# Linear attention with its key-value sums turned round: v stationary on half-array tiles, key sums on GpSimd, leftover tokens in one tile

## Chip, cores and metric

One NeuronCore of a Trainium2 chip runs the whole kernel. The metric is the device time of one execution in microseconds (us); lower is better. The engines are named as in the profile: PE (TensorE), PEld (its weight loads), DVE (VectorE), ACT (ScalarE), POOL (GpSimd) and SP (SyncE, which issues the DMAs here).

## What is computed

Three layers follow each other over 8 batches of 576 tokens. The change is in the first, an attention with a feature map and no softmax (8 heads, head dimension 64, 128 features, so 256 exponentials for each token):

```python
def phi(x):
    proj = np.einsum('bhsd,df->bhsf', x, w_phi)
    proj = proj - np.max(np.abs(proj), axis=-1, keepdims=True)
    return np.concatenate([np.exp(proj), np.exp(-proj)], axis=-1)
q_p, k_p = (phi(q), phi(k))
kv = np.einsum('bhsf,bhsd->bhfd', k_p, v)
z = np.sum(k_p, axis=2)
num = np.einsum('bhsf,bhfd->bhsd', q_p, kv)
den = np.einsum('bhsf,bhf->bhs', q_p, z)[..., None] + 1e-06
attn = num / den
```

Its output, 512 wide, goes through two more layers. `_moe_ref` mixes each token with the one before it, then computes `sigmoid(xr @ w_r) * (relu(xk @ w_k)**2 @ w_v)`, with d_ff 1024. `_moe2_ref` is `h * sigmoid(conv3(h)) @ w_out` with `h = relu(x @ w_in)`.

## The kernel before, in words

`phase_1` computes the attention and the `_moe_ref` layer and `phase_2` the last layer. The change touches `phase_1` alone.

**Pairs and batches.** Attention works on two heads at a time, a pair p of 0 to 3; head h of the pair has its 64 channels on partitions 64h to 64h+63 of `qk`. `batches` runs the program in laps: first the attention of batch 0 alone (`first_attention_steps`), then seven laps that hold the attention of batch n+1 and the MoE layer of batch n (`iteration(True, True)`), and at last the MoE layer of batch 7. In a lap the MoE layer is cut into PE tiles of 12 matmuls each, named K, R, V- and V (K- and K+ are parts of a K tile), which are put between the attention's steps.

**The order is written out by a planner.** `iteration` walks through the steps of `attention_steps`. After each one it adds that step's entry of `PE_NS` to a clock and puts in MoE tiles worth `FILL_NS` of that step. Every engine walks through the same list and does its own part of each entry, in order. No engine overtakes: what stands later on an engine's list waits for what stands before it.

**The steps of one pair**, with the lines of the profile:
- E (`features_and_keys`, PE) multiplies q and k with `phi`. q comes out with features on partitions and tokens as columns, in `ps` (or `psm`); k with tokens on partitions, in five tiles of 128 tokens for each head, the fifth with 64 tokens and 64 zeros. `shift_keys` (DVE, L750 to L758) takes each key token's largest |value| and subtracts it, into `k_shift`.
- QT (`part_maxima`, DVE, L763 to L770) makes `q_part`, the maxima of q over 32 features at a time.
- EK (`exp_k`, ACT, L643 and L645): two exponentials, `k_exp` and, in place, `k_shift`.
- M (`turn_maxima`, PE, L515) transposes `q_part`. `spread_maxima` (DVE, L774 to L782) makes `max_blocks` of it.
- KV (`sum_kv`, PE): 20 matmuls with 128 exponentials stationary and 65 columns of `v_nat` moving, 64 of v and one of ones, whose column is z. `copy_kvz` (ACT, L657) brings the result to `kvz`.
- PICK (`subtract_maxima`, PE) waits for `max_blocks` and subtracts the maxima from q's features. `exp_q` (ACT, L652) makes four exponentials `q_exp`.
- DEN and NUM (PE) give denominator and numerator. ACT copies both out (L662, L667). RC (`spread_den`, `invert`, `repeat_den`) sends the denominator through DRAM and back, and DV (`divide`, DVE, L797) writes the attention's output `x` for this pair.
- XK, HK, LK and XR, HR, LR are the mixing of `x` and its split into high and low parts, on DVE (L809, L817), ACT (L688) and DVE (L825). K, R and V tiles have parts on ACT (L672 to L677, L693) and DVE (L830, L837) too.

Most matmuls of the profile have L459, the helper `mm`; they are told apart by their tiles. A float32 matmul leaves two records, so the 20 matmuls of KV are 40 records; a transpose or a float32r matmul leaves one.

Of the kernel before, what the change touches and what calls it, by code (L numbers as in the profile page):

```python
# [11 lines left out]
P = 128  # L12
# [12 lines left out]
VW = D + 1  # L25
# [159 lines left out]
def phase_1(nc, ctx, q, k, v, w_phi, mu_k, mu_r, w_k, w_v, w_r, y_scr, den_scr, w_in):  # L185
# [56 lines left out]
    zeroed, ident_ready, pick_made, pick_ready = sem("zeroed"), sem("ident_ready"), sem("pick_made"), sem("pick_ready")  # L242
    part_zeroed, own_made, tail_zeroed, banks_zeroed, x_zeroed = sem("part_zeroed"), sem("own_made"), sem("tail_zeroed"), sem("banks_zeroed"), sem("x_zeroed")
# [11 lines left out]
    kv_summed, kvz_copied = sem("kv_summed"), sem("kvz_copied")  # L255
# [29 lines left out]
    Q0, K_TAIL, Q_MAX, Q1 = 0, BANK + D, BANK + D + 2 * F, 2 * BANK - D  # L285
    CHUNKS = (((0, BANK), (BANK, S)), ((0, D), (D, S)))
# [60 lines left out]
    def _(sp):  # L347

        def load_qk(p, a):
# [3 lines left out]
            sp.dma_start(qk[:, p % 2, 0, 0:S], q[off, p] if reg is None else q[reg + off, p]).then_inc(q_loaded[p % 2], 16)  # L353
            await_(sp, k_projected, PAIRS, a, p - 1)
            sp.dma_start(qk[:, p % 2, 1, 0:S], k[off, p] if reg is None else k[reg + off, p]).then_inc(k_loaded[p % 2], 16)

        def load_v(p, a):
# [82 lines left out]
    def _(pool):  # L440
        nc.gpsimd.memset(v_nat[:], 0.0).then_inc(zeroed, 1)
# [10 lines left out]
        pool.wait_ge(zeroed, 1)  # L452
        nc.gpsimd.memset(v_nat[:, 0:4, :, D:D + 1], 1.0).then_inc(zeroed, 1)
        nc.gpsimd.memset(v_nat[0:TAIL, 4, :, D:D + 1], 1.0).then_inc(zeroed, 1)

    @block.tensor
    def _(pe):
# [10 lines left out]
        def features_and_keys(p, a):  # L468
# [701 lines left out]
```

## Time and profile before

| | us |
|---|---|
| median of 3 runs | 1399.35 (1394.55 to 1399.78) |
| the profiled execution's own time | 1397.19 |
| its span, first to last instruction | 1395.3 |
| busy: PE, DVE, ACT, POOL | 1333.8, 756.6, 599.2, 13.1 |

The span is the length of one profiled execution. Busy is the time in which an engine had an instruction under way. PE's matmuls are pipelined: a record's length is its latency, and what a stream of them costs is the distance from start to start.

### The profile page before, as it was taken

Reading aid. Unit: us, or ns where it says so; the run is one execution under the profiler, and the core shown is the slowest. Engines: PE = TensorE matmul, PEld = TensorE weight load, DVE = VectorE, ACT = ScalarE, POOL = GpSimd, SP = SyncE. Lnnn points to the kernel's source line nnn. Section 1 sums busy time; section 2 is a strip of 40 time slices with the busy share of each in tenths; the row PEclk is TensorE's granted clock in tenths of the full one; section 3 lists DMA queues with packets and bytes.
Section 4 is the critical chain, followed back from the end, with each engine's and each line's share of the span. In section 5 each row is a group of like instructions: output and inputs, shape, how many; then the busy total and the mean of one; then the engine's idle time right before and its main releaser. Section 6 shows DMA issues by size and latency. Waiting matters only on the chain. (4 is left out here: it accounts for less than half of the span.)

```text
span 1395.3 us, 25154 instructions
## 1 busy us (share of the span) xinstructions
PE 1333.8 (96%) x9720; PEld 1192.8 (85%) x9720; DVE 756.6 (54%) x1275; ACT 599.2 (43%) x1079; POOL 13.1 (1%) x18
## 2 busy tenths in 40 slices
PE   8779999999999999999999999998899999999998
PEld 7559898889888888888888888998798998998997
DVE  6557355545654544644565455451855755754853
ACT  3345445354353533534435344352533443533532
POOL 0000000000000000000000000000300000000000
PEclk9879999999999999999999999999999999999999
DMA  4421202202212111220221221221110110110101
GB/s 136 141 62 41 59 27 79 64 18 80 62 36 71 50 50 42 66 71 15 76 62 37 71 54 50 73 70 48 65 65 31 43 65 31 41 64 32 40 30 38
DMA packets 92657, 78.56 MB, mean 56 GB/s; under 512 B 62736, under 2 KB 71056, under 8 KB 91536
## 3 DMA queue, kind: packets, MB, share of 16 engines
q1 hardware_dynamic: 92560, 77.09, 18.4%
q8 instruction: 82, 1.34, 0.4%
q14 instruction: 15, 0.12, 0.0%
HBM read 57.75 MB, written 19.02 MB: 55 GB/s over the span
## 5 line engine op out<-in xcount | busy, mean ns | idle before, releaser
L459 PE MATMUL psm<-xk_hi,wk_hi 128*128 128x288 f32 x512 | 154.4, 302 | 14.5 <-issue 7.1
L982 PE MATMUL psh<-y_hi,win_hi 128*128 128x288 f32 x512 | 154.8, 302 | 13.4 <-ACT h L1067 9.0
L830 DVE TENSOR_TENSOR k_lo<-square,k_hi 128x288 fp32r<-128x288 f32 x128 | 58.5, 457 | 195.1 <-ACT square L677 194.8
L983 PE MATMUL psh<-y_lo,win_hi 128*128 128x288 f32 x512 | 153.1, 299 | 0.0
L459 PE MATMUL psm<-k_hi,wv_hi 128*128 128x288 f32 x512 | 152.8, 299 | 0.0
L984 PE MATMUL psh<-y_hi,win_lo 128*128 128x288 f32 x512 | 152.5, 298 | 0.0
L459 PE MATMUL psm<-xk_lo,wk_hi 128*128 128x288 f32 x512 | 152.2, 297 | 0.0
L459 PE MATMUL psm<-k_lo,wv_hi 128*128 128x288 f32 x512 | 152.0, 297 | 0.0
L459 PE MATMUL psm<-xk_hi,wk_lo 128*128 128x288 f32 x512 | 151.9, 297 | 0.0
L459 PE MATMUL psm<-k_hi,wv_lo 128*128 128x288 f32 x512 | 151.7, 296 | 0.0
L1125 DVE SCALAR_TENSOR_TENSOR conv<-h,taps,conv 128x576 f32<-128x576 f32 x64 | 55.2, 862 | 143.2 <-ACT conv L1069 143.2
L459 PEld LDWEIGHTS psm<-xk_hi,wk_hi 128*128 128x128 f32 x512 | 97.5, 190 | 18.2 <-issue 12.8
L982 PEld LDWEIGHTS psh<-y_hi,win_hi 128*128 128x128 f32 x512 | 98.0, 191 | 16.2 <-ACT h L1067 11.4
L984 PE MATMUL pso<-wout_hi,g_lo 128*128 128x512 f32 x256 | 101.1, 395 | 0.0
L982 PE MATMUL pso<-wout_hi,g_hi 128*128 128x512 f32 x256 | 101.0, 395 | 0.0
L983 PE MATMUL pso<-wout_lo,g_hi 128*128 128x512 f32 x256 | 101.0, 394 | 0.0
L672 ACT ACTIVATE relu<-psm 128x288 f32<-128x288 f32 x128 | 52.1, 407 | 108.6 <-PE psm L459 108.6
L459 PEld LDWEIGHTS psm<-k_hi,wv_hi 128*128 128x128 f32 x512 | 97.3, 190 | 1.3
L983 PEld LDWEIGHTS psh<-y_lo,win_hi 128*128 128x128 f32 x512 | 98.1, 192 | 0.3
L984 PEld LDWEIGHTS psh<-y_hi,win_lo 128*128 128x128 f32 x512 | 98.3, 192 | 0.0
L1067 ACT ACTIVATE h<-psh 128x576 f32<-128x576 f32 x64 | 41.8, 653 | 131.3 <-DVE gated L1113 92.8
L459 PEld LDWEIGHTS psm<-xk_lo,wk_hi 128*128 128x128 f32 x512 | 97.4, 190 | 0.6
(130 smaller groups left out, 2900.4 us busy)
## 6 DMA issues: line engine op xcount, KB each, us to landing
v_nat<-in_v SPq DMA_DIRECT2D x32, 320.0 KB, 3.6
qk<-in_q SPq DMA_DIRECT2D x32, 288.0 KB, 3.3
qk<-in_k SPq DMA_DIRECT2D x32, 288.0 KB, 3.7
den<-den_scr SPq DMA_DIRECT2D x64, 144.0 KB, 3.0
y_scr<-y SPq DMA_DIRECT2D x64, 144.0 KB, 2.0
y<-y_scr SPq DMA_DIRECT2D x8, 1152.0 KB, 5.6
out<-rows SPq DMA_DIRECT2D x32, 256.0 KB, 2.0
stage<-in_moe_w_in SPq DMA_DIRECT2D x4, 512.0 KB, 3.2
```

The costliest lines, as they stand in the source:

```text
L459: return nc.tensor.matmul(o, lhsT, rhs, start=first, stop=last, skip_group_check=True)
L672: nc.scalar.activation(relu[:, i % 2, :], psm[:, UNIT["K", n, i] % 3, 0:HALF], ACT.Relu).then_inc(k_relu, 1)
L830: nc.vector.tensor_tensor(k2_lo[:, i, :], square[:, i % 2, :], k2_hi[:, i, :].bitcast(F32), ALU.subtract).then_inc(k2_lo_ready, 1)
L982: nc.tensor.matmul(o, wh, xh, start=first, stop=False, skip_group_check=True)
L983: nc.tensor.matmul(o, wh, xl, start=False, stop=False, skip_group_check=True)
L984: return nc.tensor.matmul(o, wl, xh, start=False, stop=last, skip_group_check=True)
L1067: nc.scalar.activation(two(h[:, j % 2, 1:1 + S]), psh[:, j % 2, :, 0:HALF], ACT.Relu, scale=0.5).then_inc(h_ready, 1)
L1125: nc.vector.scalar_tensor_tensor(out=conv[:, j % 2, :], in0=h[:, j % 2, 0:S], scalar=taps[:, 0, j:j + 1], in1=conv[:, j % 2, :], op0=ALU.m ...
```

## The change

KV is turned round. `v_nat` now is stationary, 64 columns of one head, and both sets of exponentials (2 x 128 columns) move; head 0 writes partitions 0 to 63 and head 1 partitions 64 to 127 of one PSUM bank. The result has v's channels on partitions, so ACT copies it to `kvt` (new `copy_kvt`), three PE transposes turn it back (new step T, `turn_kv`), and ACT copies those to `kvz`. z no longer is a 65th column: POOL adds the eight full key tiles down to two (new `sum_keys`, four adds a pair) and eight matmuls with a column of ones finish it. The 64 leftover tokens of both heads share one tile (9 tiles in place of 10), which shortens both exponentials from 1280 to 1152 columns. q's columns are cut 288/288 and 224/352 in place of 512/64 and 64/512. `exp_q` is done in two halves, head 0 at PICK, head 1 behind the new `kvz` copy at T. The planner's costs and fills are new.

```diff
-PE_NS = {"E": 2800, "M": 150, "PICK": 700, "KV": 4500, "DEN": 1200, "NUM": 2200,
+PE_NS = {"E": 2800, "M": 150, "PICK": 600, "T": 350, "KV": 3000, "DEN": 1200, "NUM": 2200,
-FILL_NS = {"E": 1600, "QT": 1600, "EK": 3200, "PICK": 3200, "NUM": 1600}
+FILL_NS = {"E": 1600, "QT": 1600, "EK": 4800, "T": 3200, "NUM": 1600}
...
-    CHUNKS = (((0, BANK), (BANK, S)), ((0, D), (D, S)))
+    CHUNKS = (((0, HALF), (HALF, S)), ((0, 2 * BANK - Q1), (2 * BANK - Q1, S)))
...
+        def sum_keys(p, a):
+            for e in range(2):
+                tiles = k_exp[:, e, 0:KEYS - 1, :].rearrange("s (g y) f -> s g y f", y=2)
+                await_(pool, k_exp_ready, 2 * PAIRS, a, 2 * p + e + 1)
+                await_(pool, z_summed, 2 * PAIRS, a, 2 * p + e)
+                nc.gpsimd.tensor_tensor(z_pairs[:], tiles[:, :, 0, :], tiles[:, :, 1, :], ALU.add).then_inc(z_paired, 1)
+                halves = z_pairs[:].rearrange("s (h x) f -> s h x f", x=2)
+                await_(pool, z_paired, 2 * PAIRS, a, 2 * p + e + 1)
+                await_(pool, kv_summed, PAIRS, a, p)
+                nc.gpsimd.tensor_tensor(z_sums[:, e, :, :], halves[:, :, 0, :], halves[:, :, 1, :], ALU.add).then_inc(z_summed, 1)
...
         def features_and_keys(p, a):
-            key_tile(0, TT - 1).then_inc(shared_bank, 1)
-            feature_chunk(1, 1, True)
-            feature_chunk(0, 0, True)
-            await_(pe, shared_bank, 3 * PAIRS, a, 3 * p + 1)
-            key_tile(1, TT - 1).then_inc(shared_bank, 1)
             key_tile(0, 0)
             key_tile(1, 0)
-            await_(pe, shared_bank, 3 * PAIRS, a, 3 * p + 2)
+            key_tail(0)
+            key_tail(1).then_inc(shared_bank, 1)
+            await_(pe, shared_bank, 2 * PAIRS, a, 2 * p + 1)
+            feature_chunk(0, 0, True)
+            feature_chunk(1, 1, True)
...
         def sum_kv(p, a):
             await_(pe, v_loaded, 16 * PAIRS, a, 16 * (p + 1))
-            for e, src in enumerate((k_exp, k_shift)):
-                await_(pe, k_exp_ready, 2 * PAIRS, a, 2 * p + e + 1)
+            await_(pe, k_exp_ready, 2 * PAIRS, a, 2 * p + 2)
+            own = [slice(D * h, D * h + D) for h in range(2)]
+            for t in range(TT - 1):
                 for h in range(2):
-                    for t in range(TT):
-                        last = mm(ps1[:, 0, VW * (2 * h + e):VW * (2 * h + e) + VW], src[:, h, t, :], v_nat[:, t, h, :],
-                                  t == 0, t == TT - 1)
+                    tile = (TT - 1) * h + t
+                    mm(kv_turned()[own[h], :, :], v_nat[:, tile, :], k_exp[:, :, tile, :], t == 0, False)
+            for h in range(2):
+                mm(kv_turned()[own[h], :, :], v_nat[own[h], KEYS - 1, :], k_exp[own[h], :, KEYS - 1, :], False, True)
+            await_(pe, z_summed, 2 * PAIRS, a, 2 * p + 2)
+            for h in range(2):
+                for e in range(2):
+                    mm(z_row(h, e), ones[:], z_sums[:, e, h, :], True, False)
+            for h in range(2):
+                for e in range(2):
+                    last = mm(z_row(h, e), ones[own[h], :], k_exp[own[h], e, KEYS - 1, :], False, True)
             last.then_inc(kv_summed, 1)
+
+        def turn_kv(p, a):
+            await_(pe, kvt_copied, PAIRS, a, p + 1)
+            for i in range(3):
+                last = nc.tensor.matmul(ps1[:, 1, P * i:P * i + P], kvt[:, P * i:P * i + P], ident[:], start=True, stop=True,
+                                        is_transpose=True, skip_group_check=True)
+            last.then_inc(kvz_turned, 1)
...
         def copy_kvz(p, a):
-            await_(act, kv_summed, PAIRS, a, p + 1)
+            await_(act, kvz_turned, PAIRS, a, p + 1)
             await_(act, attended, PAIRS, a, p)
```

**What moves on DVE.** In pair 1 of a steady lap this is DVE's list from the reciprocal of the denominator to the first step of `spread_maxima` before:

```order
L791 RECIPROCAL den_cols<-den_cols 128x9
L763 STREAM_TRANSPOSE q_turn<-ps 128x576 x2
L766 TENSOR_REDUCE q_part<-q_turn 128x2x18
L770 COPY q_part<-q_part 128x64
L817 SCALAR_TENSOR_TENSOR mix<-diff,mu,x 128x288 x4
L837 SCALAR_TENSOR_TENSOR y<-gate,psm 128x288
L797 TENSOR_TENSOR x<-num,den 128x576
L825 TENSOR_TENSOR xr_lo<-mix,xr_hi 128x864
L774 TENSOR_REDUCE q_max<-ps 128x32
```

The same stretch of DVE's list now:

```order
L843 RECIPROCAL den_cols<-den_cols 128x9
L869 SCALAR_TENSOR_TENSOR mix<-diff,mu,x 128x288 x3
L815 STREAM_TRANSPOSE q_turn<-ps 128x576 x2
L818 TENSOR_REDUCE q_part<-q_turn 128x2x18
L822 COPY q_part<-q_part 128x64
L869 SCALAR_TENSOR_TENSOR mix<-diff,mu,x 128x288
L889 SCALAR_TENSOR_TENSOR y<-gate,psm 128x288
L877 TENSOR_TENSOR xr_lo<-mix,xr_hi 128x864
L849 TENSOR_TENSOR x<-num,den 128x576
L877 TENSOR_TENSOR xr_lo<-mix,xr_hi 128x288
L889 SCALAR_TENSOR_TENSOR y<-gate,psm 128x288
L826 TENSOR_REDUCE q_max<-ps 128x32
```

Three mixes stand ahead of the transposes of q, and a second `xr_lo` and a second `y` ahead of `q_max`.

**What moves on ACT.** The exponentials of pair 1 and what stands around them before:

```order
L693 ACTIVATE gate<-psm 128x288 x3
L643 ACTIVATE k_exp<-k_shift 128x1280
L645 ACTIVATE k_shift<-k_shift 128x1280
L688 ACTIVATE xr_hi<-mix 128x864
L688 ACTIVATE xr_hi<-mix 128x288
L657 ACTIVATE kvz<-ps 128x260
L652 ACTIVATE q_exp<-ps 128x576 x4
L662 ACTIVATE den_rows<-ps 128x576
```

And now:

```order
L743 ACTIVATE gate<-psm 128x288 x2
L738 ACTIVATE xr_hi<-mix 128x864
L689 ACTIVATE k_exp<-k_exp 128x1152
L691 ACTIVATE k_exp<-k_exp 128x1152
L738 ACTIVATE xr_hi<-mix 128x288
L702 ACTIVATE kvt<-ps 128x384
L697 ACTIVATE q_exp<-ps 128x576 x2
L707 ACTIVATE kvz<-ps 128x384
L697 ACTIVATE q_exp<-ps 128x576 x2
L712 ACTIVATE den_rows<-ps 128x576
```

`xr_hi` of 864 columns, which waits for the three mixes, stands ahead of the exponentials, and the copy to `kvz` stands behind half of `q_exp`.

**What moves on PE** where no MoE tile lies between, in the attention of batch 0, from M of pair 0 into E of pair 1, before:

```order
L515 MATMUL ps<-ident,q_part 128x128
L459 MATMUL ps<-v_nat,k_exp 128x65 x10
L459 MATMUL ps<-v_nat,k_shift 128x65 x10
L459 MATMUL ps<-max_blocks,pick 128x512
L459 MATMUL ps<-max_blocks,pick 128x64 x2
L459 MATMUL psm<-phi,qk 128x128
```

And now:

```order
L544 MATMUL ps<-ident,q_part 128x128
L486 MATMUL ps<-k_exp,v_nat 64x256 x10
L486 MATMUL ps<-z_sums,ones 1x128 x4
L486 MATMUL ps<-k_exp,ones 1x128 x4
L486 MATMUL ps<-max_blocks,pick 128x288 x2
L486 MATMUL ps<-max_blocks,pick 128x224
L486 MATMUL ps<-max_blocks,pick 128x352
L578 MATMUL ps<-ident,kvt 128x128 x3
L486 MATMUL ps<-phi,qk 128x128 x2
```

The transposes stand between PICK and the next E, and the next E waits for `kvz`, which is copied behind them.

## Rows read from the trace of the kernel before

**Rows 1.** The page, engines: busy us, share of the span, instructions.

```profile
PE 1333.8 (96%) x9720; PEld 1192.8 (85%) x9720; DVE 756.6 (54%) x1275; ACT 599.2 (43%) x1079; POOL 13.1 (1%) x18
```

**Rows 2.** Busy time by stretch: length, then each engine's busy us; PEclk; DMA.

```profile
329.70:444.40 114.70, 111.54 (x902) 99.31 (x901) 59.99 (x112) 51.37 (x101) 0.00 (x0) 1.00 0.20 58
444.40:561.00 116.60, 113.48 (x903) 100.92 (x901) 59.97 (x112) 51.76 (x101) 0.00 (x0) 0.99 0.19 51
```

**Rows 3.** Groups by form, PE: busy us, mean ns; idle before.

```profile
L459 PE MATMUL ps<-v_nat,k_exp 128*128 128x65 f32 x640 | 76.8, 275 | 0.0
```

**Rows 4.** Timeline of PE, pair 0 of a lap: start, length.

```profile
444.65 0.37 PE L459 MATMUL ps<-phi,qk 64*128 64x128 f32 x1
...
454.54 0.33 PE L515 MATMUL ps<-ident,q_part 128*128 128x128 f32 x1
454.72 2.44 PE L459 MATMUL ps<-v_nat,k_exp 128*128 128x65 f32 x20
...
459.20 0.93 PE L459 MATMUL ps<-max_blocks,pick 128*128 128x512 f32 x4
459.97 0.29 PE L459 MATMUL psm<-xk_hi,wk_hi 128*128 128x288 f32 x1
...
463.24 3.25 PE L459 MATMUL ps<-q_exp,kvz 128*1 128x64 f32 x32
```

**Rows 5.** Waits, whole span: us in total, times, longest.

```profile
PE ps L459 <- DVE max_blocks L782: 12.2, 15, 5.0
PEld ps L515 <- DVE q_part L770: 6.0, 21, 0.3
```

**Rows 6.** Timeline of PE (first row) and DVE, pair 1 of a lap.

```profile
353.47 0.37 PE L459 MATMUL ps<-phi,qk 64*128 64x128 f32 x1
...
362.17 0.20 DVE L770 COPY q_part<-q_part 128x64 f32<-128x64 f32 x1
362.28 1.80 DVE L817 SCALAR_TENSOR_TENSOR mix<-diff,mu,x 128x288 f32<-128x288 f32 x4
...
364.48 0.76 DVE L797 TENSOR_TENSOR x<-num,den 128x576 f32<-128x576 f32 x1
365.15 1.05 DVE L825 TENSOR_TENSOR xr_lo<-mix,xr_hi 128x864 fp32r<-128x864 f32 x1
...
366.88 0.76 DVE L782 TENSOR_TENSOR max_blocks<-own_block,q_max_split 128x576 fp32r<-128x576 f32 x1
```

**Rows 7.** Timeline of ACT, pair 1 (first row) and pair 0.

```profile
361.32 1.28 ACT L645 ACTIVATE k_shift<-k_shift 128x1280 f32<-128x1280 f32 x1
...
454.89 0.39 ACT L672 ACTIVATE relu<-psm 128x288 f32<-128x288 f32 x1
...
455.99 0.39 ACT L672 ACTIVATE relu<-psm 128x288 f32<-128x288 f32 x1
```

**Rows 8.** Timeline of PE and DVE, pair 3 of a lap.

```profile
516.46 0.37 PE L459 MATMUL ps<-phi,qk 64*128 64x128 f32 x1
...
530.44 0.76 DVE L782 TENSOR_TENSOR max_blocks<-own_block,q_max_split 128x576 fp32r<-128x576 f32 x1
```

**Rows 9.** Timeline of POOL and DVE in the last layer.

```profile
977.85 0.82 DVE L1128 SCALAR_TENSOR_TENSOR conv<-h,taps,conv 128x576 f32<-128x576 f32 x1
...
981.60 2.42 POOL L1093 TENSOR_TENSOR wout_lo<-stage,wout_hi 128x1024 fp32r<-128x1024 f32 x1 [0.65 <-ACT wout_hi L1038]
...
981.60 3.02 DVE L1128 SCALAR_TENSOR_TENSOR conv<-h,taps,conv 128x576 f32<-128x576 f32 x1
```

**Rows 10.** Busy time of two stretches around PICK of pair 1; columns as rows 2.

```profile
480.00:483.40 3.40, 2.70 (x23) 2.52 (x23) 3.02 (x7) 0.39 (x1) 0.00 (x0) 1.00 0.13 43
483.40:486.80 3.40, 3.40 (x15) 3.30 (x15) 0.00 (x0) 2.28 (x4) 0.00 (x0) 0.50 0.42 96
```

**Rows 11.** Timeline of ACT, batch 0, pair 0.

```profile
22.06 0.39 ACT L657 ACTIVATE kvz<-ps 128x260 f32<-128x260 f32 x1 [3.14 <-PE ps L459]
...
23.29 2.26 ACT L652 ACTIVATE q_exp<-ps 128x576 f32<-128x576 f32 x4
```

More of the change, by code:

```diff
@@ L49, in attention_steps @@
 def attention_steps():
-    return [(s, p) for p in range(PAIRS) for s in ("E", "QT", "EK", "M", "KV", "PICK", "DEN", "NUM")]
+    return [(s, p) for p in range(PAIRS) for s in ("E", "QT", "EK", "M", "KV", "PICK", "T", "DEN", "NUM")]
 def first_attention_steps():
@@ L62, in first_attention_steps @@
         steps += [("E", p), ("QT", p), ("EK", p)] + before("DEN", "NUM") + [("WARM", p)] + before("RC")
-        steps += [("M", p), ("KV", p), ("PICK", p)] + before("DV")
+        steps += [("M", p), ("KV", p), ("PICK", p), ("T", p)] + before("DV")
     p = PAIRS - 1
@@ L213, in phase_1 @@
     max_blocks = sb_att("max_blocks", [P, TOK, 32], F32R)
-    k_shift = sb_att("k_shift", [P, 2, TT, F])
-    k_exp = sb_att("k_exp", [P, 2, TT, F])
-    pick_f = k_exp[:, :, 0, :]
+    k_exp = sb_att("k_exp", [P, 2, KEYS, F])
+    z_pairs, z_sums = sb_att("z_pairs", [P, 4, F]), sb_att("z_sums", [P, 2, 2, F])
+    pick_f = k_exp[:, 0, 0:2, :]
     q_exp = sb_att("q_exp", [P, 2, 2, S])
-    kvz = sb_att("kvz", [P, 2, 2, VW])
+    kvt = sb_att("kvt", [P, 3 * F])
+    kvz = sb_att("kvz", [P, 3, P])
     num = sb_att("num", [P, S])
@@ L283, in second_of @@
         return reg is None and off == 1
-    Q0, K_TAIL, Q_MAX, Q1 = 0, BANK + D, BANK + D + 2 * F, 2 * BANK - D
-    CHUNKS = (((0, BANK), (BANK, S)), ((0, D), (D, S)))
+    K_TAIL, Q0 = 0, BANK - HALF
+    Q1 = Q0 + S
+    Q_MAX = Q1 + S
+    CHUNKS = (((0, HALF), (HALF, S)), ((0, 2 * BANK - Q1), (2 * BANK - Q1, S)))
     def att_psum(p, a):
@@ L450, in _, with work @@
                                     pattern=[[-1, TOK]], channel_multiplier=1).then_inc(own_made, 1)
-        pool.wait_ge(zeroed, 1)
-        nc.gpsimd.memset(v_nat[:, 0:4, :, D:D + 1], 1.0).then_inc(zeroed, 1)
-        nc.gpsimd.memset(v_nat[0:TAIL, 4, :, D:D + 1], 1.0).then_inc(zeroed, 1)
+        def sum_keys(p, a):
[8 more added lines that the diff above has]
+                nc.gpsimd.tensor_tensor(z_sums[:, e, :, :], halves[:, :, 0, :], halves[:, :, 1, :], ALU.add).then_inc(z_summed, 1)
+        def work(m, a, steps):
+            if a is not None:
+                for p in range(PAIRS):
+                    sum_keys(p, a)
+        batches(pool, work)
     @block.tensor
@@ L545, in sum_den @@
                         row = 32 * (2 * h + e)
-                        mm(q_cols(1, p, a)[row:row + 1, cols], kvz[:, h, e, D:D + 1], q_exp[:, e, h, cols], True, True)
+                        mm(q_cols(1, p, a)[row:row + 1, cols], kvz[:, 2, row:row + 1], q_exp[:, e, h, cols], True, True)
         def attend(p, a):
@@ L553, in attend @@
                     for h in range(2):
-                        last = mm(q_cols(0, p, a)[D * h:D * h + D, cols], kvz[:, h, e, 0:D], q_exp[:, e, h, cols], e == 0, e == 1)
+                        last = mm(q_cols(0, p, a)[D * h:D * h + D, cols], kvz[:, e, D * h:D * h + D], q_exp[:, e, h, cols], e == 0, e == 1)
             last.then_inc(attended, 1)
@@ L608, in work @@
                     sum_kv(step[1], a)
+                elif kind == "T":
+                    turn_kv(step[1], a)
                 elif kind == "DEN":
@@ L701, in work @@
                 elif kind == "PICK":
-                    exp_q(step[1], a)
+                    exp_q(0, step[1], a)
                 elif kind == "KV":
+                    copy_kvt(step[1], a)
+                elif kind == "T":
                     copy_kvz(step[1], a)
+                    exp_q(1, step[1], a)
                 elif kind == "NUM":
```

90 lines of the change are left out of this document (50 added, 40 removed).

## The prediction

> **What bounds the kernel now.** I read the page's busy shares first: PE is busy 96% of the span [rows 1], so a change is worth what it takes off PE's list, less what it adds to PE's waits. Then busy time by stretch. The seven laps that hold attention are alike; an undisturbed one takes 114.7 us, and two of the seven take 116.6 [rows 2]. Then PE's timeline in one lap. From M on, KV's 40 records take 4.48 us (454.72 to 459.20), PICK 0.77, two MoE tiles 3.27 (so 1.6 us a tile), DEN and NUM together 3.25 with the latency of the last record [rows 4]. A record of KV is 275 ns long [rows 3] but the next starts 0.11 us later: it has 65 columns moving and 128 stationary, and the pace is that of the weight load. Last, the waits: PICK waited for `max_blocks` 15 times in `ps`, 12.2 us in all, and M for `q_part` 21 times by 0.3 us [rows 5]. So the maxima of q already end as late as KV in half of the pairs. What the change does to that chain counts as much as what it does to KV.
>
> **KV on PE.** DEN and NUM have the new form (32 or 64 columns of the array, two or four matmuls side by side). They send 1728 columns one after another (576 for DEN, 1152 for NUM) in about 3.05 us net of the last latency, 1.77 ns a column [rows 4]. New KV sends 4 x 256, then 256 for the leftover tile, then 128 and 128 for z: 1536 columns, 2.7 us, and I add 0.2 for changes of form: 2.9 in place of 4.48. PICK loses its two narrow matmuls: 0.6 in place of 0.77. T adds three transposes, each a record like M's, which is 0.18 us ahead of KV [rows 4]: 0.40. DEN and NUM have more even chunks: -0.05. E has a new exposed wait on its own tails and shorter tails: 0, with 0.1 either way. So PE's own list gets 1.6 + 0.15 - 0.4 + 0.05 = 1.4 us shorter for each pair. The bounds for KV are 2.7 (no change of form costs anything) and 3.9 (below).
>
> The Trainium skill (TensorEngine Tiling, Tiling Modes, Key Properties) says that a change of tiling mode, not of tile alone, drains the engine. New KV changes its tile shape five times between M and PICK. By the rows such a step costs 0.1 or so; by the rule, priced with the 275 ns of a record, KV would be 3.9 us. That would show only in pair 3, where KV ends last, and make the time some 6 us longer.
>
> **The chain of the maxima.** It decides when PICK can start. I walk DVE's new list from the start of E. Before, PICK starts 14.55 us after E in pair 0 [rows 4], 14.2 in pair 1 (366.88 + 0.76 - 353.47, [rows 6]) and 14.7 in pair 3 [rows 8]; pair 2 is bound by KV as pair 0 is, with one tile less: 14.1. Now every pair has one more MoE tile between E and M, so M is 1.25 to 1.6 later.
> - Pair 0: the added tile is K7. Its ACT part queues behind the exponentials, and K tiles go through ACT at 1.10 us each (454.89 to 455.99, [rows 7]); its `k_lo` stands ahead of `q_max`. `max_blocks` ends at 15.4.
> - Pair 1: three mixes (0.43 us each, 4 in 1.80, [rows 6]) now stand ahead of the transposes of q, so `q_part` ends 1.5 later, at 10.4. Then one mix, `y`, `xr_lo` 1.0, `x` 0.7, `xr_lo` 0.4, `y` 0.4, and 1.5 from `q_max` to the end of `max_blocks`: 15.2. The exponentials now wait for `xr_hi`, which waits for the mixes; they end at 10.8 (before: 361.32 + 1.28 - 353.47 = 9.1, [rows 7]).
> - Pair 2: as pair 0, with `x` in the queue: 14.95. Pair 3: only R tiles are added, no `k_lo` is ahead, and `x` waits for its denominator until about 11.5: `max_blocks` ends at 13.8, and KV at 14.0 decides.
>
> **What GpSimd does to that chain.** This is the cost that I weigh most. In the last layer a POOL op of 1024 columns takes 2.42 us, and a DVE instruction that starts with it takes 3.02 us where it otherwise takes 0.82 [rows 9]: it is held for as long as POOL works, less 0.2. The held instruction reads two tensors of SBUF, as do `k_lo`, `mix`, `xr_lo`, `x` and `max_blocks`. The new adds take 2 x (1.25 + 0.65) = 3.8 us a pair by that row, from the end of the first exponential on. In pair 0 most of it falls where DVE waits for ACT anyway: 15.5 in place of 15.4. In pair 2 it costs 0.8: 15.75. In pair 1 DVE has no slack: the adds run from 9.6 on between its ops, each holding the next one: about +2.3, 17.5. In pair 3 they are over before `x`.
>
> [...]
>
> **Sum of a lap.** PICK later by 0.95 + 3.3 + 1.65 - 0.7 = +5.2. One tile more done ahead of it in each pair: 4 x 1.6 = -6.4. Behind PICK, T less the small gains: +0.2 a pair, +0.8. At the lap's end six V tiles in place of eight R and V tiles hide the last denominator, `x` and the split; I find `xk_lo` ready just when K+ wants it: +0.1 (up to +0.8). That is -0.3 to -0.5 a lap, -3 for seven. The 2.1 us of extra length in two laps is a stretch of 3.4 us at half the clock (1.2 GHz) after PE stood still for 0.7 us behind the weight-bound KV [rows 10]; new KV keeps the array busier, and I count these as gone: -4.
>
> **Batch 0** has no tiles between steps. E of the next pair waits for `kvz`, which so far was copied before PICK (22.06, ahead of `q_exp` at 23.29, [rows 11]). Now ACT does half of `q_exp` first, 1.1 us of the 2.26 for four, then the copy, 0.4, after 0.25 for the signal; less T's own place the next E starts 1.7 us later, three times, and the last DEN 0.4: +5.3. Bounds 2 and 8; none of it can be a gain, since PICK there waits for the denominators of the pair before, not for KV whose longest wait was 5.0 us [rows 5].
>
> Against the profiled execution's own 1397.2 (2.2 below the median, within the runs' spread): 1397.2 - 3 - 4 + 5.3 = 1395.5, so **1396**, own range 1386 to 1406. What the edit takes off PE is given back as waits for `max_blocks`.
>
> **Rivals.** A measurement of this kernel tells a change from none at about 0.5%, 7 us.
> - *The adds hold nobody up.* PICK at 15.4, 15.2, 14.95, 14.0: +2.1 - 6.4 + 0.9 = -3.4 a lap. 1397.2 - 24 - 4 + 5.3 = **1375**. For it: POOL's op could be short in so small a size. Against: the held instruction of [rows 9].
> - *It does what it says.* The waits stay as they are and 1.4 us go from each of 28 pairs: -39, with batch 0: **1360**. For it: PE is 96% busy. Against: one more K tile's work on ACT and DVE stands ahead of `max_blocks`.
> - *Slower: PE cools in front of PICK 1.* With KV done at 14.1 and PICK at 17.5, PE stands still 3.4 us in each lap. After 0.7 us of standing still the granted clock was 0.50 for the next 3.4 us, which costs 1.9 [rows 2, 10]. If that follows in all seven laps where it came in two before, it adds 5 x 1.9 to 1397.2 - 3 + 5.3: **1409**. The point is a wait of some 2 us or more behind dense work; against it, waits of 0.3 to 0.6 us before PICK left the clock whole in the other laps.
>
> **Chances.** Forecast 0.45, adds harmless 0.22, as it says 0.10, cooling 0.23. The forecast's own range lies 0.15 under 1392.4, 0.28 within 0.5%, 0.02 over 1406.4; cooling 0.14 over and 0.09 within. Faster 0.47, same 0.37, slower 0.16. The range reaches from 1366 (most of the harmless case) to 1412 (most of the cooling one).
>
> **What would show it.** KV: from M to z some 2.9 us on PE. Adds: z_pairs about 1.25 us, and beside them `xr_lo` or `k_lo` longer than 2 us. PICK's wait for `max_blocks`: 1.3, 3.4, 1.8 and 0 us in pairs 0 to 3. Batch 0: E of pairs 1 to 3 waits for ACT's `kvz`. A `max_blocks` that ends before KV in pairs 0 to 2, or DVE's ops at their old lengths beside POOL, would make the forecast wrong; so would a KV over 4 us.

## The result, and the profile after

The changed kernel takes **1442.47 us** (median of 4 runs, 1440.22 to 1446.7), the kernel before beside it 1396.95 (4 runs, 1392.69 to 1399.78): ratio 1.0332, 95% interval 1.029 to 1.0374. That is 3.3% slower, and 46 us from the prediction of 1396, outside its range. The profiled execution is one of 1440.22 us; the one of before took 1397.2.

The page's busy shares of the kernel after, to be laid beside [rows 1]:

```profile
PE 1328.0 (92%) x9688; PEld 1130.2 (79%) x9688; DVE 788.8 (55%) x1274; ACT 609.0 (42%) x1111; POOL 163.3 (11%) x144
```

TensorE (PE) was busy 6 us less and its span is 43 us longer, so it stood still 49 us more; part of what is left of its busy time ran at the lower clock (below). VectorE (DVE) is 32 us busier with one instruction less; no operation was added there, so its instructions became longer.

The first four laps after; columns as [rows 2]:

```profile
113.57:236.40 122.83, 115.52 (x899) 95.87 (x898) 63.48 (x113) 52.38 (x104) 18.73 (x16) 0.93 0.16 47
236.40:354.05 117.65, 109.71 (x897) 90.83 (x897) 64.87 (x113) 52.69 (x105) 17.94 (x16) 0.99 0.17 51
354.05:474.00 119.95, 111.24 (x897) 92.04 (x897) 63.85 (x112) 52.41 (x105) 17.94 (x16) 0.97 0.17 52
474.00:593.30 119.30, 111.37 (x898) 92.41 (x898) 64.46 (x113) 53.03 (x105) 18.45 (x16) 0.97 0.18 54
```

A lap is 3 to 8 us longer than 114.7, and its clock is rarely whole. The 43 us lie so: the first lap starts at 113.6 where it started at 101.2 (batch 0, +12.4); six laps take 717.9 where they took 691.3 (+26.7); the seventh with what follows until the last layer +5.8; the last layer -1.7.

PE's timeline in pair 0 of a lap (start, length, idle before and its releaser), with E at 354.05, beside [rows 4]:

```profile
354.05 0.86 PE L486 MATMUL ps<-phi,qk 64*128 64x128 f32 x8
...
357.29 0.40 PE L486 MATMUL psm<-xk_hi,wk_hi 128*128 128x288 f32 x1
...
365.73 0.27 PE L544 MATMUL ps<-ident,q_part 128*128 128x128 f32 x1
365.93 2.53 PE L486 MATMUL ps<-k_exp,v_nat 128*64 128x256 f32 x20
368.39 0.40 PE L486 MATMUL ps<-z_sums,ones 128*1 128x128 f32 x8
368.72 0.40 PE L486 MATMUL ps<-k_exp,ones 64*1 64x128 f32 x8
370.08 0.82 PE L486 MATMUL ps<-max_blocks,pick 128*128 128x288 f32 x4 [0.97 <-DVE max_blocks L834]
370.74 0.49 PE L578 MATMUL ps<-ident,kvt 128*128 128x128 f32 x3
370.98 0.38 PE L486 MATMUL psm<-xr_hi,wr_hi 128*128 128x288 f32 x1
```

KV with z runs from 365.93 to its last start at about 368.85, 2.9 us as forecast; PICK takes 0.66 until the transposes, these 0.24 until the next tile: the edit does on PE what it says. But the first tile comes 3.24 us after E's start, where it came 2.77 after it before (444.65 to 447.42), and PICK stands 0.97 us idle.

PE's waits over the whole span, beside [rows 5]:

```profile
PE ps L486 <- DVE max_blocks L834: 32.8, 22, 4.7
PE ps L486 <- POOL z_sums L474: 15.1, 11, 1.5
PE psm L486 <- DVE xk_lo L877: 10.8, 6, 3.3
```

DVE and POOL (GpSimd) in pair 1 of the same lap, where E starts at 379.28; before: [rows 6]:

```profile
389.75 0.72 DVE L822 COPY q_part<-q_part 128x64 f32<-128x64 f32 x1
390.39 0.51 DVE L869 SCALAR_TENSOR_TENSOR mix<-diff,mu,x 128x288 f32<-128x288 f32 x1
390.82 0.44 DVE L889 SCALAR_TENSOR_TENSOR y<-gate,psm 128x288 f32<-128x288 f32 x1
391.18 1.22 DVE L877 TENSOR_TENSOR xr_lo<-mix,xr_hi 128x864 fp32r<-128x864 f32 x1
392.33 1.82 DVE L849 TENSOR_TENSOR x<-num,den 128x576 f32<-128x576 f32 x1
394.07 0.97 DVE L877 TENSOR_TENSOR xr_lo<-mix,xr_hi 128x288 fp32r<-128x288 f32 x1
...
396.08 0.76 DVE L834 TENSOR_TENSOR max_blocks<-own_block,q_max_split 128x576 fp32r<-128x576 f32 x1
```

```profile
389.12 1.29 POOL L470 TENSOR_TENSOR z_pairs<-k_exp 128x512 f32<-128x512 f32 x1 [20.84 <-ACT k_exp L689]
390.57 0.92 POOL L474 TENSOR_TENSOR z_sums<-z_pairs 128x256 f32<-128x256 f32 x1 [0.16 <-POOL z_pairs L470]
391.63 1.90 POOL L470 TENSOR_TENSOR z_pairs<-k_exp 128x512 f32<-128x512 f32 x1
393.61 1.12 POOL L474 TENSOR_TENSOR z_sums<-z_pairs 128x256 f32<-128x256 f32 x1
```

Read the two by their ends. `q_part` ends at 390.47, just behind the first `z_pairs` (390.41); `x` at 394.15, 0.62 behind an add's end (393.53); the second `xr_lo` at 395.04, 0.31 behind the next one's (394.73). `x` takes 1.82 us where it took 0.76 [rows 6]. The adds are held as well: the second `z_pairs` starts while the long `xr_lo` still runs (to 392.40) and needs 1.90 where the first needs 1.29.

`x` isn't the costliest of them over the whole run. These are VectorE's groups after (count, busy us, mean ns), then the copy in a run without adds (run 1 below):

```profile
L822 DVE COPY q_part<-q_part 128x64 f32<-128x64 f32 x32 | 21.2, 661 | 1.1
L849 DVE TENSOR_TENSOR x<-num,den 128x576 f32<-128x576 f32 x32 | 35.9, 1123 | 33.1 <-DMA den<-den_scr 32.9 <-issue 0.2
```

```profile
L821 DVE COPY q_part<-q_part 128x64 f32<-128x64 f32 x32 | 6.3, 196 | 1.1
```

The small copy alone is 14.9 us longer, `x` 11.7, `k_lo` 5.7 and `xr_lo` 4.9.

What TensorE's clock does there: the same columns for stretches of 3.4 us.

```profile
392.70:396.10 3.40, 1.34 (x22) 0.36 (x20) 3.30 (x7) 0.49 (x1) 1.95 (x2) 0.99 0.02 6
396.10:399.50 3.40, 2.60 (x11) 2.56 (x12) 0.74 (x1) 1.22 (x3) 0.00 (x0) 0.50 0.45 130
399.50:402.90 3.40, 3.40 (x16) 3.40 (x15) 0.00 (x0) 1.45 (x3) 0.00 (x0) 0.50 0.02 5
402.90:406.30 3.40, 3.40 (x36) 1.98 (x36) 0.45 (x1) 0.00 (x0) 0.00 (x0) 1.00 0.13 43
```

PE is busy for 1.34 of 3.40 us while it waits for `z_sums` and then `max_blocks`; the clock is then at 1.2 GHz (0.50) for 6.8 us, with 11 and 16 instructions, and 36, of another mix, in the next stretch at the whole clock. From the start of the first lap to that of the seventh 44 us pass at 0.50, before the change 10.

### The profile page after: what moved, and what is told of

The parts are those of the page before. It is cut to its first block and busy times, and to the rows that moved or that the text cites. A ratio compares the mean times of both kernels' runs of the same rounds, so it can differ in the third digit from the quotient of the medians.

```text
span 1438.4 us, 25420 instructions
## 1 busy us (share of the span) xinstructions
PE 1328.0 (92%) x9688; PEld 1130.2 (79%) x9688; DVE 788.8 (55%) x1274; ACT 609.0 (42%) x1111; POOL 163.3 (11%) x144
## 5 line engine op out<-in xcount | busy, mean ns | idle before, releaser
L486 PE MATMUL psm<-xk_hi,wk_hi 128*128 128x288 f32 x512 | 159.7, 312 | 21.2 <-DVE xk_lo L877 10.8
L470 POOL TENSOR_TENSOR z_pairs<-k_exp 128x512 f32<-128x512 f32 x64 | 91.6, 1432 | 762.8 <-ACT k_exp L689 758.2
L486 PE MATMUL psm<-k_hi,wv_hi 128*128 128x288 f32 x512 | 157.2, 307 | 0.0
L486 PE MATMUL psm<-xk_lo,wk_hi 128*128 128x288 f32 x512 | 156.1, 305 | 0.0
L882 DVE TENSOR_TENSOR k_lo<-square,k_hi 128x288 fp32r<-128x288 f32 x128 | 64.3, 502 | 118.2 <-ACT square L727 118.2
L486 PEld LDWEIGHTS psm<-xk_hi,wk_hi 128*128 128x128 f32 x512 | 101.3, 198 | 28.6 <-issue 18.6
L889 DVE SCALAR_TENSOR_TENSOR y<-gate,psm 128x288 f32<-128x288 f32 x64 | 28.7, 449 | 137.8 <-PE psm L486 137.2
L486 PE MATMUL ps<-phi,qk 64*128 64x128 f32 (+1 forms) x632 | 91.0, 309 | 11.6 <-DVE pick L790 6.3
L486 PEld LDWEIGHTS psm<-xk_lo,wk_hi 128*128 128x128 f32 x512 | 101.4, 198 | 0.0
L486 PEld LDWEIGHTS psm<-xk_hi,wk_lo 128*128 128x128 f32 x512 | 101.1, 198 | 0.0
```

What stands on the lines that cost most here:

```text
L470: nc.gpsimd.tensor_tensor(z_pairs[:], tiles[:, :, 0, :], tiles[:, :, 1, :], ALU.add).then_inc(z_paired, 1)
L486: return nc.tensor.matmul(o, lhsT, rhs, start=first, stop=last, skip_group_check=True)
L882: nc.vector.tensor_tensor(k2_lo[:, i, :], square[:, i % 2, :], k2_hi[:, i, :].bitcast(F32), ALU.subtract).then_inc(k2_lo_ready, 1)
L889: nc.vector.scalar_tensor_tensor(out=y[:, i % 2, :], in0=gate[:, i, :], scalar=1.0, in1=psm[:, UNIT["V", n, i] % 3, 0:HALF], op0=ALU.add, ...
```

## The experiments

After the result I had this theory: the adds on GpSimd hold VectorE back, so PICK waits, and PE's clock falls behind the longer waits; E and batch 0 add their own. Each is tried apart. Runs 1 to 7 are one execution each, and so is the first time of run 9; the kernel before, executed with them, took 1396.5 us beside runs 1 to 4 and 1393.8 beside runs 5, 6, 7 and 9. Such a time is compared below with the fastest execution of the changed kernel, 1440.2, unless it says otherwise; executions of one kernel here differ by 5 to 8 us. An idle matmul is one whose result nobody reads.

**1. No adds at all** (`e1_no_adds`). `z_sums` is set to ones once, so the key sums lack all but the leftover tokens; nobody waits for GpSimd.

```diff
-                for p in range(PAIRS):
-                    sum_keys(p, a)
+                pass
...
-            await_(pe, z_summed, 2 * PAIRS, a, 2 * p + 2)
```

> The changed kernel with GpSimd's four adds a pair left out: z_sums is filled with ones once and nobody waits for it, so z is wrong; every matmul stays. Theory H (the adds hold VectorE's instructions, so max_blocks is late): in pair 1 of a steady lap max_blocks ends at 15.2 to 15.6 us after the start of E in place of 17.6, in pair 2 at 15.3 in place of 16.3, in pair 0 hardly earlier; k_lo and xr_lo return to their old lengths (0.46 and 1.05 us); a lap is 2.5 to 3 us shorter by that alone, and most of the eleven half-clock stretches of the laps go with the shorter waits: 1405 to 1415 us in all. Rival W (only TensorE's wait for z_summed costs): max_blocks ends where it did, pair 1 still has PICK at 17.6, and the time stays over 1430.

Measured: 1403.05 us. DVE in pair 1 (E at 366.44):

```profile
376.91 0.20 DVE L821 COPY q_part<-q_part 128x64 f32<-128x64 f32 x1
...
377.82 1.05 DVE L876 TENSOR_TENSOR xr_lo<-mix,xr_hi 128x864 fp32r<-128x864 f32 x1
378.79 0.75 DVE L848 TENSOR_TENSOR x<-num,den 128x576 f32<-128x576 f32 x1
379.45 0.45 DVE L876 TENSOR_TENSOR xr_lo<-mix,xr_hi 128x288 fp32r<-128x288 f32 x1
...
380.94 0.76 DVE L833 TENSOR_TENSOR max_blocks<-own_block,q_max_split 128x576 fp32r<-128x576 f32 x1
```

The same instructions are back at 0.20, 1.05, 0.75 and 0.45. `max_blocks` ends 15.83, 15.25, 15.43 and 14.21 us after E in pairs 0 to 3, with the adds 15.98, 17.56, 16.25 and 14.73. Without the adds the kernel is 37 us shorter (1405 to 1415 us was expected); a lap takes 114.3, and from the first lap to the start of the seventh 14 us pass at 0.50 in place of 44.

**2. Adds made, nobody waits for them** (`e7_adds_unread`). The adds run as in the changed kernel; PE multiplies a constant tile, so the key sums again lack most tokens. PE's wait for `z_sums` goes, VectorE's hold stays. So that nothing is overwritten, ScalarE and VectorE wait for the adds in PE's place, at the next exponentials and at `x` (not shown).

```diff
-            await_(pe, z_summed, 2 * PAIRS, a, 2 * p + 2)
...
-                    mm(z_row(h, e), ones[:], z_sums[:, e, h, :], True, False)
+                    mm(z_row(h, e), ones[:], z_fixed[:, e, h, :], True, False)
```

> The changed kernel with the adds made as before, but TensorE reads a constant in place of their result and doesn't wait for them, so z is wrong. Theory H: VectorE is held as before, max_blocks ends at 17.6 us in pair 1, the time is within 5 us of the changed kernel's 1440 us. Rival W (TensorE's wait for the sums is what costs): the time falls to that of the run without adds.

Measured: 1441.49 us, as slow as the changed kernel's 1440 to 1447. `max_blocks` ends 15.98, 17.56, 16.25 and 14.74 us after E, to 0.01 us as with the wait. The wait for `z_sums` (15.1 us in the table of waits) costs nothing that can be told: PICK behind it waits longer for the maxima, 54.2 us in all where it was 38.3. It is the hold.

**3. The changed kernel kept busy** (`e4_warm`). 23 idle matmuls of the identity in each lap, put where PE waits in pairs 0 to 2.

```diff
+            for _ in range({0: 4, 1: 6, 2: 7}.get(p, 0) if not first_of(a) else 0):
+                mm(ps1[:, 1, 0:P], ident[:], ident[:], True, True)
             await_(pe, blocks_ready, PAIRS, a, p + 1)
```

(and 6 more in pair 1 ahead of the wait for `z_sums`.)

> The changed kernel with 23 idle matmuls of 128 columns a steady lap put where TensorE stands still (6 ahead of the wait for the sums and 6 ahead of PICK in pair 1, 7 ahead of PICK in pair 2, 4 in pair 0); they write a bank that nobody reads. Theory C (part of the loss is the half clock that follows the long waits): most of the eleven half-clock stretches in the laps (each 3.4 us long, some 1.7 us lost) go, and the kernel is 10 to 18 us faster: 1422 to 1430. Rival (the clock doesn't matter, the waits are the whole loss): no faster than 1437, or slower by the matmuls themselves, where a wait was shorter than they are.

Measured: 1427.12 us, 13 less, with the maxima where they were. The third and fourth lap, columns as [rows 2]:

```profile
354.44:471.58 117.14, 114.04 (x944) 94.82 (x943) 64.14 (x112) 52.73 (x106) 18.53 (x16) 1.00 0.17 47
471.58:589.34 117.76, 115.23 (x943) 96.30 (x943) 64.50 (x112) 52.47 (x104) 17.94 (x16) 0.99 0.19 53
```

PE does some 46 records more than in the same laps above and is done 2.8 and 1.5 us sooner, while the clock reads 1.00 and 0.99 where it read 0.97. So some 13 of the 43 us are clock, and that is a lower bound: from the first lap to the start of the seventh 20 us still pass at 0.50, where it was 44, and 10 before the change.

**4. Tails earlier inside E** (`e3_e_order`).

```diff
             key_tile(0, 0)
-            key_tile(1, 0)
             key_tail(0)
             key_tail(1).then_inc(shared_bank, 1)
+            key_tile(1, 0)
+            key_tile(0, 1)
+            key_tile(1, 1)
             await_(pe, shared_bank, 2 * PAIRS, a, 2 * p + 1)
             feature_chunk(0, 0, True)
             feature_chunk(1, 1, True)
-            key_tile(0, 1)
-            key_tile(1, 1)
```

> The changed kernel with another order inside E: the two 64x64 tails second to fourth and three more key tiles behind them, so that the wait for their bank is covered by key tiles before q's first chunks. Theory E (the exposed wait and the changes of tile form make E 3.14 us from first to last start, 0.47 more than before): E falls to 2.8 to 2.9 us, and 32 of them give 8 to 12 us: 1428 to 1433. Rival (E is hidden behind VectorE's chain to PICK, so its length is free): E is shorter and the time stays within 3 us of 1440.

Measured: 1438.99 us, 1.2 below the fastest run of the changed kernel, above the 1428 to 1433 that I expected and within the rival's 3 us. From its first to its last instruction (by their starts) E takes 2.89 us in place of 3.03, half of what I expected; before the change it took 2.57. The rival's reason doesn't hold all the same: `max_blocks` and PICK come 0.14 us earlier behind the start of E in pairs 0 to 2, and an undisturbed pair is 0.13 to 0.14 us shorter (pair 0: 25.10 for 25.24). Over 32 pairs that is 4 us; in this execution 51 us of the six laps ran at 0.50 where it was 44, which takes about as much. So the place of the tails is less than a third of E's 0.46; the rest lies in the form of its other instructions (chunks of 288, 288, 352 and 224 columns among the tiles in place of 512 and 64, narrow tails), which I didn't separate.

**5. The key sums on TensorE** (`f1_z_on_pe`), correct arithmetic with no adds: 16 narrow matmuls a pair in place of 4.

```diff
-            await_(pe, z_summed, 2 * PAIRS, a, 2 * p + 2)
-            for h in range(2):
-                for e in range(2):
-                    mm(z_row(h, e), ones[:], z_sums[:, e, h, :], True, False)
+            for t in range(TT - 1):
+                for h in range(2):
+                    for e in range(2):
+                        mm(z_row(h, e), ones[:], k_exp[:, e, (TT - 1) * h + t, :], t == 0, False)
```

> The changed kernel with GpSimd's adds given back to TensorE: z sums all eight full key tiles with 16 matmuls of 128 columns, four side by side, in place of 4 of the added-up tiles; GpSimd does nothing in the laps. By the run without adds (1403.05 us, laps of 114.2), and 0.65 us more of matmuls a pair, which only pair 3 and part of pair 0 show since PICK comes later than KV in the others: 1403 to 1412 us. If the adds' price were something else than VectorE being held (memory traffic of GpSimd, the wait), this would tell nothing new; if it is above 1425, the extra matmuls are on the path in all pairs and the account of the waits is wrong.

Measured: 1406.75 us. All key sums by PE cost 3.7 us more than leaving them out (one execution each, within the spread of executions), the adds on GpSimd 36 us more than this (median against this time). Four narrow matmuls lie side by side in different columns of the array: their records start 0.007 us apart. PE is busy 22 us more than in run 1 (1336.5 for 1314.1): in pair 3, where no maxima are waited for, PICK comes 0.66 us later (15.25 for 14.59), in pairs 0 to 2 where it came before. The extra work fills PE's wait for the maxima and is nearly free for that reason.

**6. Batch 0's copy first** (`f2_kvz_first`): version 5, and in batch 0 `kvz` is copied ahead of the exponentials of q.

```diff
-                elif kind == "PICK":
+                elif kind == "PICK" and not first_of(a):
                     exp_q(0, step[1], a)
...
                     copy_kvz(step[1], a)
+                    if first_of(a):
+                        exp_q(0, step[1], a)
```

> The kernel with z on TensorE, and in batch 0 alone the copy to kvz ahead of both halves of q_exp on ScalarE. Theory B (in batch 0 the next E waits for kvz, which stands behind half of q_exp): E of pairs 1, 2 and 3 starts 1.1 us earlier after PICK each, and with the half clock it sits in up to twice that: the first lap starts 3 to 6 us earlier than in the run with z on TensorE, the laps stay. Rival: E is held by something else (the loads, num_copied) and nothing moves.

Measured: 1399.80 us, 7 below version 5; the first lap starts at 109.6 in place of 113.6, and the other 3 us are within the spread of executions. ACT's rows of the changed kernel, batch 0, pair 0, beside [rows 11], show what was undone:

```profile
23.07 0.49 ACT L702 ACTIVATE kvt<-ps 128x384 f32<-128x384 f32 x1 [4.07 <-PE ps L486]
23.45 1.05 ACT L683 ACTIVATE wk_hi<-mix 128x1024 fp32r<-128x1024 f32 x1
24.40 1.18 ACT L697 ACTIVATE q_exp<-ps 128x576 f32<-128x576 f32 x2
25.46 0.50 ACT L707 ACTIVATE kvz<-ps 128x384 f32<-128x384 f32 x1
```

A piece of weights (`wk_hi`, 1.05 us) also stands ahead of the copy of `kvz`. I hadn't counted it. This run leaves it where it is. E of the next pair starts at 26.0, before at 22.7.

**7. One tile later** (`f3_late_tile`): version 5 with `"EK": 3200, "T": 4800`, one MoE tile from ahead of M to behind the transposes.

> The kernel with z on TensorE and the planner's fill before M at 3200 ns as in the kernel before, with the tile put behind T (4800). My account: in each pair M comes 1.57 us earlier, but max_blocks only 0.4 to 1.2 us earlier (its K tile's work on ScalarE and VectorE is 1.1, one y is 0.4), so a pair gets 0.4 to 1.1 us longer where max_blocks decides: laps 1 to 3 us longer, 1410 to 1420. Rival F (the table that puts one more tile ahead of M is part of the loss): laps 1 to 3 us shorter, under 1403.

Measured: 1428.09 us, 21 slower than version 5 and 8 above what I expected. In pairs 0 and 3 PICK comes 1.0 to 1.2 us earlier, in pairs 1 and 2 0.4, for a tile of 1.6 that now lies behind it: PE waits for the maxima instead. In pairs 1 and 2 M isn't what delays them most; that it is VectorE's own queue is my reading of the rest.

**8. One tile earlier** (`h2_early_tile`): version 9 below with `"EK": 6400, "T": 1600`, and the copy of `kvz` first in every batch.

> The last version (key sums on TensorE, no adds, tails earlier in E, idle matmuls in batch 0), with one MoE tile moved from behind the transposes to ahead of M, and ScalarE's copy for kvz first in every batch. Theory (TensorE waits 0.2 to 1.0 us for the maxima ahead of PICK, and VectorE's own queue, not M, sets when they are ready): a tile of 1.6 us ahead of M moves PICK by about 0.9, and kvz is ready 1.5 us after the transposes, so DEN follows the one tile left there with 0.1 to 0.3 of waiting: 0.4 us less for each of 28 pairs, 1392 - 11 = 1381 us. Rival (the maxima move with M as they did when the tile was moved the other way, by 1.1 us in pair 0): PICK is 1.1 to 1.6 later and the wait for kvz is added, 1392 to 1400 us.

Measured: 1436.18 us (4 runs; ratio 1.0282, 1.0263 to 1.0301). I expected 1381, the rival 1392 to 1400: both missed. PE and, below, ACT in pair 1 (E at 375.3):

```profile
391.98 0.81 PE L485 MATMUL ps<-max_blocks,pick 128*128 128x288 f32 x4
392.67 0.55 PE L579 MATMUL ps<-ident,kvt 128*128 128x128 f32 x3
395.96 2.27 PE L485 MATMUL ps<-q_exp,kvz 128*1 128x224 f32 x24 [1.16 <-ACT q_exp L700]
```

```profile
393.25 0.49 ACT L710 ACTIVATE kvz<-ps 128x384 f32<-128x384 f32 x1 [0.64 <-PE ps L579]
393.64 2.27 ACT L700 ACTIVATE q_exp<-ps 128x576 f32<-128x576 f32 x4
```

PICK no longer waits here, but DEN does: I had costed its wait by `kvz` and forgotten the four exponentials of q (2.27 us), which DEN needs too. Over the span PE waits for them 28 times, 33.9 us in all, which is most of the 43 us that this costs over version 9. PICK is 1.3 to 1.6 us later behind E in pairs 1 to 3, as the rival had it, and 2.5 later in pair 0 (18.23 for 15.73). With two tiles behind the transposes DEN doesn't wait for `q_exp` in the laps, with one it does.

**9. All of it** (`f4_all`): version 6 with E's order of run 4, and idle matmuls in PE's waits of batch 0 (18 ahead of PICK of pairs 1 and 2, 6 behind the transposes). `i1_all_again` is the same kernel, timed; `i2_no_warm` has no idle matmuls.

> z on TensorE, the copy to kvz first in batch 0, the other order inside E, and in batch 0 idle matmuls where TensorE stands still (18 before PICK of pairs 1 and 2, 6 behind T). By the parts: 1403 to 1410 less 3 to 6 (kvz) less 4 (E) less 3 to 6 (full clock in batch 0): 1388 to 1400, as fast as the kernel before or slightly faster. If it stays above 1405, batch 0's length is not a matter of clock and copies.

> The version that ran once at 1392.2 us, timed: the changed kernel with the key sums on TensorE (no adds), ScalarE's copy for kvz ahead of the exponentials of q in batch 0, the tails earlier in E, and idle matmuls in batch 0. One theory: its single time stands for it, 1392 within 2, and a ratio to the kernel before of 0.997. Rival: that run was a good one (the granted clock was whole in six of the seven laps), and its median lies at 1394 to 1398, no faster than before.

> The same without the idle matmuls of batch 0. In the version with the copy first alone (1399.8) batch 0 had 37 us of half clock and E took 5.4 us there, and the first attention lap began at 109.6; with the tails earlier and the idle matmuls at 103.4. Theory (the idle matmuls did it): without them the lap begins at 108.5 to 109.5, and the time is 1397 to 1399. Rival (in batch 0 VectorE's queue is the bound, as the kernel before with idle matmuls suggests, whose lap began no earlier for them: 103.4 against 101.2): the lap begins at 104 to 106 and the time is 1393 to 1395.

Measured: 1392.17 in one execution; timed again, **1393.6** (12 runs, 1391.24 to 1396.67) against 1395.46 for the kernel before (23 runs), ratio 0.9987, interval 0.9972 to 1.0001. Without the idle matmuls 1396.81 (10 runs), ratio 1.0009, interval 0.9993 to 1.0024. The first lap starts at 103.4 and 104.5 with them, at 109.7 without. So in this kernel they give 3 us (their means are 3.0 apart, with an interval of 1.2 to 4.8), and the whole edit, freed of what it cost, is worth nothing that can be told. In the profiled executions six laps take 686.6 us where they took 691.3 before the change, and the first starts 3.3 later.

The page of `i1_all_again`:

```profile
PE 1334.2 (96%) x10564; PEld 1141.2 (82%) x10564; DVE 749.6 (54%) x1274; ACT 609.2 (44%) x1111; POOL 12.5 (1%) x16
```

VectorE is at 749.6 us, 39 below the changed kernel (run 1, without the adds, has 749.7): that much of its busy time was the hold.

**10. The control** (`h1_before_warm`): the kernel before, with idle matmuls in batch 0 alone.

```diff
+            for _ in range(16 if first_of(a) and p in (1, 2) else 0):
+                mm(ps1[:, 1, 0:P], ident[:], ident[:], True, True)
             await_(pe, blocks_ready, PAIRS, a, p + 1)
```

(and 3 behind PICK of pairs 0 to 2.)

> The kernel before, with nothing of the change, and idle matmuls (128x128) in TensorE's waits of batch 0 alone: 16 ahead of PICK of pairs 1 and 2, 3 behind PICK of pairs 0 to 2. It asks whether the last version's gain (1392.2 us with the key sums on TensorE, ScalarE's copy first, the tails earlier in E and idle matmuls in batch 0) owes anything to the change. Theory (it owes nothing, what was gained there is the clock of batch 0, which the kernel before can have as well): half-clock stretches of batch 0 go from 31 us in all to some 15, E of batch 0 takes 2.6 us where it took 4.2, and 1396 - 7 = 1389 us. Rival (the change's form of KV keeps its own advantage, the clock of batch 0 matters little in the kernel before): 1396 within 2, above the 1392 of that version.

Measured: 1400.47 us (10 runs; ratio 1.0027, 1.0012 to 1.0043), 4 us slower than the kernel before, where I expected 1389 and the rival 1396. Its clock rose (0.97 over batch 0, before 0.86), E took 2.57 us there where it took 4.2, and the first lap still began 2.2 us later. PE's waits of its first 110 us:

```profile
PE psm L459 <- DVE xk_lo L829: 9.5, 2, 6.2
```

What the clock gave comes back as a wait for `xk_lo` (before 5.2 us in all). I read this as VectorE's work setting the length of batch 0, not PE's; no run moved that work, so it is argued and not shown.

## Why the prediction was wrong, step by step

Per lap PICK is later by 1.5, 3.4, 2.2 and 0 us in pairs 0 to 3, where "PICK later by 0.95 + 3.3 + 1.65 - 0.7" stood. The mechanism that the forecast weighed most, the hold by GpSimd, was right. What failed are four terms of its sum: the length of E (put at 0), the lap's end, the clock (counted as a gain) and batch 0.

- **KV, PICK, T on PE: right.** 2.9, 0.66 and 0.24 us by starts, where 2.9, 0.6 and 0.40 stood. The ten matmuls of 256 columns (20 records) with their change of form fit in 2.46 us; where the form changes inside KV the next start comes 0.31 us later in place of 0.22, so about 0.1 a change. The Trainium skill (TensorEngine Tiling, Key Properties) says that a change of tiling mode drains the engine. If it does here, the drain costs that 0.1 and not a record's 0.275 (priced so, five changes on 2.7 would be 4.1; the prediction's 3.9 is a slip).
- **The chain of the maxima: right within 0.4.** 15.4 / 15.2 / 14.95 without the hold; without adds, run 1 has 15.83 / 15.25 / 15.43, of which 0.46 is E. Less that, pairs 0 and 2 are met; pair 1 is 14.8, and the 15.2 that stood there fitted only because the missing E made up for it.
- **The hold by GpSimd: right in mechanism and size, and the rival "harmless" fell.** Forecast 0.1, 2.3 and 0.8 us; the difference to run 1 is 0.15, 2.3 and 0.8. The sign that I gave for it, an `xr_lo` or `k_lo` of over 2 us, didn't come: the longest are 1.22 and 0.82, and the longest `x` is 1.82. Only what is left of the add counts: no `k_lo` started with more than 0.51 us of an add to go, no `x` with more than 1.20. `y`, with one operand in PSUM, kept its 0.44 us and the reductions theirs, but the copy of `q_part`, with one input and that in SBUF, took 0.72 in place of 0.20, and over the run it is the largest part of the hold, 14.9 of 39 us; I had not counted it. The Trainium skill (SBUF — State Buffer, Who interferes with whom) says that a copy can enter a mode that takes the ports shared with GpSimd, and that a reduction on trn2 never contends. The trace agrees: the copies that started under an add took 0.68 us or more, the nine reductions their usual time.
- **E: the step that failed first.** "0, with 0.1 either way" is +0.46 us by its starts, in every pair at the whole clock. It shifts the chain of the maxima too, since all of it is counted from E: 1.9 us a lap, 13 us over seven laps. I had costed the columns, not the narrower tails and the waits inside the step (run 4 gave 0.14 of it back, in E and in PICK behind it).
- **The lap's end: too small.** "+0.1 (up to +0.8)" for `xk_lo` is 1.1: from NUM 3's end to the next E 17.4 us with six V tiles, 22.7 before with eight V and two R tiles of 1.6 (the prediction says "eight R and V tiles"; its -6.4 takes the four right). Over the six laps it is 0.6 to 2.2. In the lap above `x` waits for the denominators' load, and K+ for `xk_lo`:

```profile
469.90 0.76 DVE L849 TENSOR_TENSOR x<-num,den 128x576 f32<-128x576 f32 x1 [1.43 <-DMA den<-den_scr]
```

```profile
472.90 0.37 PE L486 MATMUL psm<-xk_hi,wk_hi 128*128 128x288 f32 x1 [0.77 <-DVE xk_lo L877]
```

- **The clock: the rival came true on top.** "-4, I count these as gone" is about +13 (run 3). The forecast held that a busier KV keeps the clock whole; it falls behind the waits ahead of PICK (44 us at 0.50 with them, 14 without in run 1, 20 with them filled in run 3), and I had myself forecast 3.4 us of such a wait. The two parts of the prediction contradicted each other.
- **Batch 0: +12.4 where "+5.3" stood**, above the bound of 8. The copy of `kvz` behind `q_exp` was seen; a weight piece ahead of both wasn't, nor that E there takes 4.4 to 5.4 us, most of it at the lower clock (before: 2.6 to 4.2). (The terms that stood there, 1.7 three times and 0.4, make 5.5, not 5.3.) Copy first gives 4 back at the first lap's start (run 6), the idle matmuls 5 (run 9).

In sum, over the forecast's 1395.5: E 13, the lap's end 7, the clock 17 (the 13 and the 4 that were to go), batch 0 7. That makes 44, and the profiled run is 1440.2. The terms for E and the lap's end are one lap's numbers times seven and the clock's is run 3's, so the close fit is in part luck. The adds, which I had priced directly at 3.2 us a lap, make some 23 us that the sum held; I put the rest of the 37 us of run 1 down to the clock that their waits cost, which goes with its 30 us less at 0.50.

What stays open: which part of E's new form costs the 0.3 us that its order doesn't (no run gave E its old form back, so its 13 us are counted from the trace and not tested), and why idle matmuls that raise the clock of batch 0 in both kernels bring the first lap forward in one alone.

## What to carry to other kernels

Before work goes to an idle engine, look at who shares its way to memory: 151 us of adds on GpSimd took 39 us of VectorE and, with the clock, 37 of the kernel. When work leaves the bound engine, ask first what it will wait for next; here PE already waited up to 1 us for the maxima in 12 of the 24 pairs of six laps, so a PE list shorter by 1.4 us a pair could gain next to nothing, and the version without the hold gained 0.8 us a lap. And a step that is only rearranged has a price: read the order of matmuls inside it as closely as the ones that are removed.

## What the runs showed of the hardware that I had not expected

- The hold works in both directions, for whichever engine comes second: `z_pairs` took 1.29 us undisturbed and 1.90 behind `xr_lo`.
- It lasts to the end of the add and no longer. Single records of the changed kernel: each held `x` ends 0.61 to 0.62 us behind the end of the add that it started under, each held `k_lo` 0.31 to 0.32, each held copy of `q_part` 0.05 to 0.06. Undisturbed they take 0.76, 0.46 and 0.20, so all three end their own length less 0.14 behind the add, and one that started less than 0.14 before the add's end lost nothing.
- A copy within SBUF of 64 columns was held (0.72 us in place of 0.20), and 32 of them are the largest part of what VectorE lost, 14.9 of 39 us. The small cast of `q_max` was held too where it started under an add (0.39 us or more in place of 0.18).
- Idle matmuls are no cure by themselves: in the changed kernel's laps they gave 13 us, in batch 0 of version 9 they gave 3, and in batch 0 of the kernel before they gave nothing (it was 0.3% slower with them).
- Key sums as 1-column matmuls, four side by side, kept TensorE busy for 22 us more and cost 3.7 us of the kernel's time (run 5 less run 1), a tenth of what GpSimd's adds cost.
